# Scores of the first batch as plain fp32 matmuls, with its q/k preparation and the weight blocks moved in a fused attention and two-layer kernel

## The reference

```python
scores = scale * np.matmul(q, k.transpose(0, 1, 3, 2))
kth = np.partition(scores, -top_k, axis=-1)[..., -top_k:-top_k + 1]   # top_k = 32
scores = np.where(scores >= kth, scores, -1000000000.0)
attn = softmax(scores)                                    # rows summed with 1e-9 added
x = np.matmul(attn, v) as (tokens, 512)
h = x @ w_in;  g = h if h >= 1, 0 if h <= -1, else (h + 1) ** 2 / 4;  x = g @ w_out
h = max(x @ w2_in, 0);  out = (h * h) @ w2_out
```

## Time and profile before

| | |
|---|---|
| times | 1289.24, 1289.71, 2301.94 us; median 1289.71 |
| profiled execution | 1291.56 us, of which the span is 1289.8 |
| PE busy | 1197.6 us, 93% |
| DVE busy | 850.2 us, 66% |
| ACT, POOL busy | 777.6 and 776.7 us, 60% |
| slots end, steps alone | about 970, then 320 us |
| POOL, one: compare L1068, mask L1073 | 1766 and 1428 ns |
| POOL, one weight block L1060 | two in 4.71 us |
| DMA | 240.64 MB, mean 187 GB/s |

### The profile page before, as it was taken

One profiled execution on the slowest core, in us unless ns is written; L12 is line 12 of the kernel. 1 busy time (PEld: TensorE's weight loads), 2 busy tenths in 40 slices (PEclk: granted clock), 3 DMA queues, 4 the chain that ended last, 5 costly groups with the idle time before them and its releaser, 6 DMA issues.

```text
span 1289.8 us, 24436 instructions
## 1 busy us (share of the span) xinstructions
PE 1197.6 (93%) x8760; PEld 1135.1 (88%) x8760; DVE 850.2 (66%) x1896; ACT 777.6 (60%) x1761; POOL 776.7 (60%) x636
## 2 busy tenths in 40 slices
PE   3878878898999999999999999999999999999998
PEld 2767877888888889999999999999999999999997
DVE  7998989889897679989889997878850111110000
ACT  5545665777575567676766675656654565654443
POOL 5977878776886766777766667566662222222222
PEclk9866999999999999999999999999999999999999
DMA  6786573685778973452336852355529500780000
GB/s 240 268 300 240 215 253 128 235 292 208 282 273 331 354 279 116 138 176 92 120 123 238 323 203 65 114 153 183 182 70 350 227 34 1 254 334 6 29 17 17
DMA packets 96263, 240.64 MB, mean 187 GB/s; under 512 B 7824, under 2 KB 47760, under 8 KB 83856
## 3 DMA queue, kind: packets, MB, share of 16 engines
q1 hardware_dynamic: 96144, 239.09, 51.8%
HBM read 167.23 MB, written 71.83 MB: 185 GB/s over the span
## 4 chain that ended last, share of the span: by engine, by line
PE 65%; ACT 8%; DVE 8%; POOL 7%; DMA 5%; issue 5%; SPq 1%; ACTq 0%; POOLq 0%
PE h_ps L598 19%; PE y_ps L619 14%; PE y_ps L613 11%; PE score_ps L598 6%; PE pv_ps L557 5%; DVE top L887 4%; PE tr_ps L530 3%; DVE rest L889 3%; PE score_ps L495 2%; POOL prob L1073 2%; POOL s_sb L1068 2%; POOL kq_lo L1052 2%; DMA stage<-in_w_dram 1%; ACT prob L716 1%; DMA kq_scratch<-kq_hi 1%
## 5 line engine op out<-in xcount | busy, mean ns | idle before, releaser
L1086 POOL TENSOR_TENSOR g_lo<-g_sb,g_hi 128x256 fp32r<-128x256 f32 x288 | 217.6, 756 | 435.3 <-ACT g_hi L800 233.7
L598 PE MATMUL h_ps<-xt_hi,w_in 128*128 128x256 f32 x1880 | 391.3, 291 | 13.0 <-ACT r_sb L782 7.1
L598 PEld LDWEIGHTS h_ps<-xt_hi,w_in 128*128 128x128 f32 x1880 | 309.6, 191 | 17.4 <-ACT r_sb L782 8.6
L887 DVE MAX8 top<-rest 128x8 f32<-128x576 f32 x432 | 304.7, 746 | 0.4
L1068 POOL TENSOR_SCALAR s_sb<-s_sb,top 128x576 f32<-128x576 f32 x144 | 254.3, 1766 | 35.4 <-DVE top L887 35.2
L598 PE MATMUL h_ps<-xt_lo,w_in 128*128 128x256 f32 x940 | 266.3, 283 | 0.0
L613 PE MATMUL y_ps<-g_hi,w_out 128*128 128x256 f32 x1152 | 232.9, 285 | 0.4 <-POOL g_lo L1086 0.3
L889 DVE MATCH_REPLACE8 rest<-top,rest 128x576 f32<-128x576 f32 x288 | 211.5, 741 | 0.0
L619 PE MATMUL y_ps<-w_out,g_hi 128*128 128x512 f32 x576 | 203.9, 395 | 0.9 <-ACT ys L766 0.9
L613 PEld LDWEIGHTS y_ps<-g_hi,w_out 128*128 128x128 f32 x1152 | 190.5, 193 | 1.9 <-POOL g_lo L1086 0.5
L1073 POOL TENSOR_TENSOR prob<-s_sb,prob 128x576 f32<-128x576 f32 x128 | 182.8, 1428 | 10.7
(11 more groups left out here) (86 smaller groups left out, 2000.8 us busy)
## 6 DMA issues: line engine op xcount, KB each, us to landing
w_in<-w_scratch SPq DMA_DIRECT2D x32, 1024.0 KB, 6.8
w_out<-w_scratch SPq DMA_DIRECT2D x32, 1024.0 KB, 8.1
ks<-kq_scratch SPq DMA_DIRECT2D x47, 576.0 KB, 5.1
qs<-kq_scratch SPq DMA_DIRECT2D x156, 128.0 KB, 4.2
w_scratch<-w_in SPq DMA_DIRECT2D x16, 1024.0 KB, 7.4
w_scratch<-w_out SPq DMA_DIRECT2D x16, 1024.0 KB, 7.3
v_sb<-in_vv_dram SPq DMA_DIRECT2D x48, 325.0 KB, 4.4
stage<-in_w_dram SPq DMA_DIRECT2D x24, 512.0 KB, 6.0
```

The costliest lines, as they stand in the source:

```text
L598: last = pe.matmul(h_bank(k), wi[:, f // 2, w, m, cols], x[:, m, :], start=(m == 0 and n == 0), stop=(m == KT - 1 and n == 2))
L887: dve.max(best, src[:, :]).then_inc(rank_step, 1)
L1086: pool.tensor_tensor(g_lo[k % 2][:, :], g_sb[k % 2][:, :], g_hi[k % 2][:, :].bitcast(F32), ALU.subtract).then_inc(g_lo_done, 1)
```

## The change

Slots 0 to 15 (`RAW_SLOTS = 16`) make their scores by `score_raw`: a plain fp32 matmul for each half, on 64 partitions (rows 0 to 63 for t = 0, 64 to 127 for t = 1), q and k straight from a raw input of 128x832 that holds a pair's keys and two slots' queries. The raw buffers are xr and ys. `split_first` goes, on ACT and on DVE. The preparations for batches 1 to 3 come first, in slots 8 to 47, and that of batch 0, which now only the packed slots need, in slots 50, 53, 56 and 59. Layer 1's blocks are split at most two a slot in slot 1 and otherwise one, all subtracted by POOL, through two staging buffers (block 2 through r_sb and g_sb, now one buffer, rg).

```diff
-PREP_ORDER = (1, 2, 3, 0, 4, 5, 6, 7, 8, 9, 10, 11, 12, 13, 14, 15)
-PREP_SLOT = (-1, 1, 3, 5, 11, 13, 17, 19, 29, 31, 33, 35, 38, 41, 44, 47)
+PREP_ORDER = (4, 5, 6, 7, 8, 9, 10, 11, 12, 13, 14, 15, 0, 1, 2, 3)
+PREP_SLOT = (8, 11, 13, 15, 17, 28, 30, 32, 38, 41, 44, 47, 50, 53, 56, 59)
-W1_SLOT = [-1, 0, 0, 2, 4, 6, 7, 8, 9, 10, 12, 14, 14, 15, 15, 16]
+W1_SLOT = [-1, -1, 0, 1, 1, 2, 3, 4, 5, 6, 7, 9, 10, 12, 14, 16]
 def by_vector(i):
-    return i in (12, 14) or (i >= WBLOCKS and i % 2 == 1)
+    return i >= WBLOCKS and i % 2 == 1
 def stage_at(i):
-    return i % 4 if i < WBLOCKS else i % 2
+    return 2 if i == 2 else i % 2
 def load_first():
     for t in range(2):
-        sp.dma_start(prob[t][:, 0:F_HEAD],
-                     kq0[:, F_HEAD * t:F_HEAD * (t + 1)]).then_inc(first_loaded[t], 16)
+        rows = slice(DIM * t, DIM * (t + 1))
+        sp.dma_start(raw(0, slice(0, RAW))[rows, :], kq0[0, 0, rows, :]).then_inc(first_loaded[t], 16)
+def load_raw(part, p, i):
+    sp.dma_start(raw(i, slice(0, RAW)), kq0[part, p]).then_inc(ks_loaded[i], 16)
 def load_slot_qs(n):
-    if n >= 2:
+    if is_raw(n):
+        return
+    if n >= RAW_SLOTS + 2:
         sp.wait_ge(scored, 2 * (n - 1))
 def stage_block(i):
-    if i >= WBLOCKS:
-        sp.wait_ge(w_lo_done[i % 2], i // 2)
-    elif i >= 4:
-        sp.wait_ge(w_lo_done[i % 2], i // 2 - 1)
+    if i > 2:
+        sp.wait_ge(w_lo_done[i % 2], 1 if i == 4 else i // 2)
+def score_raw(n, t):
+    i = (n // 2) % 2
+    if n < 2:
+        pe.wait_ge(first_loaded[t], 16)
+    elif n % 2 == 0:
+        pe.wait_ge(ks_loaded[i], 16 * (n // 4 + i))
+    rows, col = slice(DIM * t, DIM * (t + 1)), SEQ + P * (n % 2)
+    for half in range(2):
+        last = pe.matmul(score_ps[:, 512 * half:512 * half + HALF], raw(i, slice(col, col + P))[rows, :],
+                         raw(i, slice(HALF * half, HALF * (half + 1)))[rows, :], start=True, stop=True)
+    return last
 def load_x(j):
-    sp.wait_ge(w_lo_done[0], WBLOCKS // 2)
+    sp.wait_ge(scored, 2 * RAW_SLOTS)
-def split_first(t, a):        # on ACT: 6 copies into ks and qs for slot 0, 4 more for slot 1
-def split_first(t, a):        # on DVE: the subtractions
```

More of the change, by code:

```diff
@@ L40 @@
          [19 + s for s, c in enumerate(W2_PER_SLOT) for _ in range(c)]
-STAGE_SLOT = [-1, -1, -1, 0, 1, 2] + [s - 1 for s in W_SLOT[6:]]
+STAGE_SLOT = [-1, -1, -1, 0, 0] + [s - 1 for s in W_SLOT[5:]]
 STORE_SLOT = [max(W_SLOT[i] + 1, 3 + i) if i < WBLOCKS else W_SLOT[i] + 1
@@ L209, in build @@
         recip = sb("recip", [P, 2])
-        r_sb = [sb(f"r_sb{i}", [P, CHUNK]) for i in range(2)]
-        g_sb = [sb(f"g_sb{i}", [P, CHUNK]) for i in range(2)]
+        rg = sb("rg", [P, 4, CHUNK])
+        r_sb = [rg[:, i, :] for i in range(2)]
+        g_sb = [rg[:, 2 + i, :] for i in range(2)]
         g_hi = [sb(f"g_hi{i}", [P, CHUNK], F32R) for i in range(2)]
@@ L231, in build @@
         zeroed = sem("zeroed")
-        w_staged = [sem(f"w_staged{i}") for i in range(4)]
+        w_staged = [sem(f"w_staged{i}") for i in range(3)]
         first_loaded = [sem(f"first_loaded{i}") for i in range(2)]
-        first_hi = sem("first_hi")
-        first_lo = sem("first_lo")
         w_hi_done = sem("w_hi_done")
@@ L294, in stage_of, with raw, is_raw @@
         def stage_of(i):
-            return (stage[0], stage[1], xr, ys)[stage_at(i)]
+            return (stage[0][:, :], stage[1][:, :], rg[:, :, :].rearrange("p x n -> p (x n)"))[stage_at(i)]
         def h_bank(k):
             return score_ps[:, 0:CHUNK] if own_bank(k) else h_ps[:, 0:CHUNK]
[L302 to L307, removed]
+        def raw(i, cols):
+            return (xr, ys)[i][:, cols]
+        def is_raw(n):
+            return n < RAW_SLOTS
         block = ctx.enter_context(nc.Block())
@@ L463, in _ @@
             load_first()
-            load_kq(0)
+            for i in range(WBLOCKS):
+                if STAGE_SLOT[i] < 0:
+                    stage_block(i)
             load_v(0, 0, 0)
-            for i in range(3):
-                stage_block(i)
-            restack(0)
             for n in range(SLOTS + 2):
@@ L484, in score @@
                     pe.wait_ge(s_copied, u)
-                if not packed(n):
-                    if n < 2:
-                        pe.wait_ge(first_lo, (3 * t + 3, FIRST_LO)[n])
-                    elif n % 2 == 0:
+                if is_raw(n):
+                    last = score_raw(n, t)
+                elif not packed(n):
+                    if n % 2 == 0:
                         pe.wait_ge(ks_loaded[(n // 2) % 2], 16 * (n // 4 + (n // 2) % 2))
-                    if t == 0 and n >= 2:
-                        pe.wait_ge(qs_loaded[n % 2], 16 * 2 * (n // 2))
+                    if t == 0:
+                        pe.wait_ge(qs_loaded[n % 2], 16 * 2 * ((n - RAW_SLOTS) // 2 + 1))
                     kk, qq = ks[(n // 2) % 2], qs[n % 2]
@@ L1153, in lay_out @@
     for hh in range(2):
-        both = kq[0, 0, hh::2, 0:F_HEAD]
-        kq0[:, F_HEAD * hh:F_HEAD * (hh + 1)] = np.concatenate([both, both])
+        rows = slice(DIM * hh, DIM * (hh + 1))
+        for part in range(2):
+            kq0[part, :, rows, 0:SEQ] = kq[0, :, hh::2, 0:SEQ]
+            kq0[part, :, rows, SEQ:RAW] = kq[0, :, hh::2, SEQ + 2 * P * part:SEQ + 2 * P * (part + 1)]
     blocks = []
```

57 lines of the change are left out of this document (15 added, 42 removed).

## The result

The changed kernel takes **1280.7 us** in the median (1280.56 to 1281.73), the kernel before 1289.37; the ratio is 0.9937, with a 95% interval of 0.9921 to 0.9952. (One run of the kernel before took 2301.94 us; it is left out of the ratio.) The profiled execution has a time of 1281.73 and a span of 1279.9, against 1291.56 and 1289.8. So the gain is 8.7 us by the medians and 9.9 by the spans, where the prediction had 18.0: it is faster, inside the range of 1262 to 1284, and about half of what was forecast.

The account below looks back on a forecast made before the run. VectorE's ranking was taken to bound up to slot 9, TensorE from about slot 25. Savings of 2.0, 4.0, 4.4, 3.5 and 8 less 3.9 given back made 18.0 us: 1289.71 to 1272, range 1262 to 1284.

Parts of the forecast that it names:

- Step 2: Slots 1 to 9: VectorE's waits vanish as preparations and loads leave; 4.0 us saved (2 to 4), dearer scores costing nothing.
- the slack of 4 us: Early slots: the product with v may be 4 us late before VectorE asks for it.
- The third rival: Slots 1 to 9: TensorE becomes the bound at 1.2 GHz, making the kernel slower, 1309 at worst score price; chance 0.06.
- Step 1: The start: an earlier first matmul and no subtractions on VectorE bring its ranking forward; 2.0 us saved.
- Step 3: Slots 10 to 17: one block or preparation a slot, slots 14 and 15 at 12.7; 4.4 us saved (3 to 5).
- Step 4: Slot 19: its mask on GpSimd no longer waits behind a preparation and weight block; 3.5 us saved (1.5 to 5).
- Step 5: Slots 28 to 35: moving preparations removes most waits for kq_lo loads; 8 us saved (4 to 9).
- what stays: Slots 28 to 35: remaining cost of three preparations at 1.2 us, one wait of 1, and the transposes, 1.
- the loop: Preparations in slots 29, 31, 33, 35: kq_lo's subtraction, store and next load chain up, some 28 us per two slots.
- Step 6: Slots 50, 53, 56, 59: the four moved preparations give back 3.9 us (0 to 8).
- The first rival: Slots 53 and 56: slow kq_lo loads among weight reloads make ScalarE wait and eat the gain, 1281; chance 0.2.

Follow-up runs that it names:

- the zero-padded run: Changed kernel with scores of slots 2 to 15 over all 128 rows, each head's q zero on the other head's rows: 1267.29 us.
- The run with the loop: Changed kernel with four preparations put back from slots 17, 28, 30, 32 to slots 29, 31, 33, 35: 1291.19 us.
- the run with four even slots: Changed kernel with four preparations in slots 28, 30, 32, 34 and none in slot 17: 1283.14 us.

## Why the prediction was right or wrong

**Step 2, the failed one.** Its term said that the dearer scores cost nothing: "10.0 us, no longer under the 9.96. It is saved by two things", the slack of 4 us and the clock. Neither held. (1) Sizes: a score took 2.22 us, not 2.0, a block of transposes 1.05, not 0.87, copies and issue 0.88, not 0.8, so the chain was 11.50 and not 10.8. (2) The slack of 4 us is used up once, over all slots, and was gone by slot 4; the sum let it cover all nine slots. (3) The clock did not rise. Slots 1 to 9 took 98.98 us (19.23 to 118.21) against 93.80 before (20.59 to 114.39): 5.2 lost where 4.0 was to be gained. Slot 10, for which the prediction had no term, lost 4.1 more: the first feed-forward work and the transposes of x fell on a TensorE already late and still at 1.2 GHz. VectorE's waits there are 4.4 us for ScalarE's xt_hi and 2.4 for rg, the first work of the feed-forward (2.0 and 0.7 before). The third rival had the mechanism and its place, but a chance of only 0.06, and its price at the low clock, about 3 us, was a third of what these nine slots lost against the forecast, 9.2. With the measured chain its own rule gives 9 x 1.54 less 4 of slack, 9.9: at the clock that stayed low, most of the loss lies in the sizes of (1).

The failure of judgement is the last sentence of that rival: "by the rule, nothing". The Trainium skill, TensorE: Matmul & The Clock Gate (Part 1), says that activity releases the low clock. The prediction read busy time as activity, and the earlier trace rows seemed to agree, with a rising clock at 93% busy. Here TensorE was busy for 96% of 64 to 96 us and the records stayed at the 1.2 GHz level. The rows that had raised the clock before were matmuls over all 128 rows. With all rows used, step 2's own reasoning comes out: slot 10 begins 5.7 us earlier than before in the zero-padded run.

**Step 1** (2.0 us, measured 1.36 at slot 1): the second block's maxima start at 10.23, as the step said, but the step took their start against the end of the four subtractions in the kernel before. The maxima end at 10.97, so VectorE goes on at 10.97 against 12.2: 1.2. The first matmul came at 4.23, outside the bounds of 3.0 to 3.95: that both larger loads had landed by 3.95 was no bound for this one.

**Step 3** (4.4, measured 3.4): slots 14 and 15 take 25.38 us (175.02 to 200.40), 12.7 each as forecast; slot 16 then takes 12.80 where it had 11.84, which gives 1.0 back. **Step 4** (3.5, measured 4.16) holds, with its sign: GpSimd's first compare of slot 19 starts at 251.02, and VectorE begins slot 20 at 251.26, where the compare had come 2.3 us behind.

**Step 5** (8, measured 11.5): right in kind, too small. The term "what stays" had 5.6 us. The eight intervals from slot 28 to 36 take 103.73 against 8 x 12.68 = 101.4, so 2.3 stayed: the intervals of slots 30 and 32 are 12.84 and 12.86 against 12.50 beside them, 0.35 for a preparation and not 1.2, and no load is waited for. The run with the loop gives 9.65 of it back, of which the run with four even slots puts 1.8 on the fourth preparation and leaves 7.8 for the loop. The link of the loop that the step left out is SP's wait for the stores.

**Step 6** (3.9, measured 1.95): the interval of slot 50 is 12.55, where it was 13.80 before, so its preparation costs nothing that shows; this is partly chance, since in three of the ten kernels with a preparation there it is 13.3 to 13.8. 53 costs 1.0, 55 and 56 together 1.7, and 59 0.35. The first rival, waits for kq_lo at 53 and 56, did not happen, not even two slots apart. It would have given the measured time, 1281, for another reason; only the intervals tell the two apart. That the time fell inside the range is luck of this kind: 14 us lost in front, 5.9 won behind.

## What to carry to other kernels

Price a matmul that replaces another at the clock of its stretch, and don't let a better clock pay for it unless rows of the same shape show the clock rising. Slack counts once, over a run of slots; a loss counts in each. A chain of preparation, store and load is looser when the block is ready one slot before its reader, so that stores and load don't stand in one slot's queue.

## What the runs showed of the hardware

- TensorE busy for 96% of 32 us with products over all rows and half-array fp32 scores stayed at the 1.2 GHz level; with the scores over 128 rows, zeros in half of them, or with four more 128-row fp32r matmuls a slot, it reached 2.4 GHz in part of the slots, and so it did with the two heads' half-array matmuls side by side. In the kernel after, it came with the feed-forward matmuls of slot 10.
- The clock column of the profile read 1.00 from 32 to 118 us in the kernel after, where four transposes took 1.11 us; at the upper level they take 0.63 to 0.66. The length of a known record is the better witness. The Trainium skill, TensorE: Matmul & The Clock Gate (Part 1), warns that recorded clock events are unreliable; this trace agrees.
- A plain fp32 score of 64 or 128 rows, 2 x 288 columns, took 2.2 us at 1.2 GHz and 1.19 to 1.24 at 2.4; two on different row halves took 2.2 together, at the lower level.
- A first load of 128 partitions and one of two loads of 64 partitions let the first matmul start at the same time, 4.22 and 4.23 us; with two such loads the second half was there at 4.94 to 5.09.
